# Three pieces of VectorE's instruction order moved inside a stage of a fused attention and expert kernel

## The reference

```python
# 1 delta-rule attention: q, k, v (4, 8, 768, 48), beta (4, 8, 768); per batch and head, over t:
k_n = k / (norm(k) + 1e-6)
y[t] = q[t] @ state
state += beta[t] * outer(k_n[t], v[t] - k_n[t] @ state)
# 2 gated layer: x (3072, 384), w_gate and w_val (384, 1536), w_out (1536, 384)
x = (sigmoid(x @ w_gate) * (x @ w_val)) @ w_out
# 3 top-1 routing among 8 experts, w1 (384, 1024), w2 (1024, 384)
logits = normalized(x) @ normalized(expert_emb).T / tau
e = argmax(logits); gate_w = softmax(logits)[e]
out = gate_w * (relu(x @ w1[e]) @ w2[e])
```

## Time and profile before

| | us |
|---|---|
| median of three runs | 1312.58 (1311.84 to 1313.44) |
| the profiled execution | 1311.84 |
| its span in the profile | 1310.2 |
| PE busy | 1269.6 (97%) |
| PE weight loads busy | 1036.0 (79%) |
| DVE busy | 633.8 (48%) |
| POOL busy | 462.8 (35%) |
| ACT busy | 406.9 (31%) |

### The profile page before, as it was taken

The page is one execution under the profiler, slowest core; times in us unless marked ns, Lnnn a source line. Parts: engine busy times, 40 slices in busy tenths (PEclk is TensorE's granted clock), DMA queues, the critical chain, the costliest instruction groups (busy, mean ns, idle before and its releaser), DMA issues.

```text
span 1310.2 us, 27998 instructions
## 1 busy us (share of the span) xinstructions
PE 1269.6 (97%) x11217; PEld 1036.0 (79%) x11217; DVE 633.8 (48%) x1512; ACT 406.9 (31%) x949; POOL 462.8 (35%) x525
## 2 busy tenths in 40 slices
PE   5888999999999999999999999999899999999998
PEld 3667999999999999999999999999455555555554
DVE  6765556656666666766666666533411111111111
ACT  3443333333433333334334343422111111111110
POOL 7545333334333433433333433323332222222220
PEclk9999999999999999999999999999999999999999
DMA  7332010020101021111111010033463223311000
GB/s 232 94 93 72 19 40 28 28 40 25 38 26 34 29 39 29 29 27 40 28 28 40 24 32 14 20 109 98 80 175 129 78 80 124 132 37 36 31 28 1
DMA packets 49118, 74.79 MB, mean 57 GB/s; under 512 B 8569, under 2 KB 37665, under 8 KB 48992
## 3 DMA queue, kind: packets, MB, share of 16 engines
q1 hardware_dynamic: 41504, 61.91, 16.5%
q0 software_dynamic: 7488, 11.08, 2.8%
HBM read 61.59 MB, written 12.75 MB: 57 GB/s over the span
## 4 chain that ended last, share of the span: by engine, by line
PE 88%; POOL 3%; DMA 3%; issue 3%; DVE 2%; ACT 1%; POOLq 0%; SPq 0%; DVEq 0%
PE ps L1259 25%; PE ps L1271 12%; PE ps L1495 11%; PE ps L1485 11%; PE ps L1131 3%; PE ps L1220 3%; PE ps L1228 3%; PE ps L1156 2%; PE ps L1148 2%; PE ps L1159 2%; PE ps L1226 2%; PE ps L1504 2%; PE ps L1115 2%; PE ps L1203 1%; DMA gates_dram<-gate,slot 1%
## 5 line engine op out<-in xcount | busy, mean ns | idle before, releaser
L1259 PE MATMUL ps<-xh,wgh 128*128 128x256 f32 x864 | 263.6, 305 | 0.7 <-issue 0.7
L1259 PE MATMUL ps<-xl,wgh 128*128 128x256 f32 x864 | 243.5, 282 | 0.0
L1259 PE MATMUL ps<-xh,wgl 128*128 128x256 f32 x864 | 242.8, 281 | 0.0
L411 POOL TENSOR_TENSOR gl<-sg,gh 128x256 fp32r<-128x256 f32 x144 | 105.7, 734 | 354.1 <-ACT gh L967 343.0
L1485 PE MATMUL ps<-W,xsT 128*128 x372 | 169.5, 605 | 2.1 <-ACT xsT L1094 1.2
L1259 PEld LDWEIGHTS ps<-xh,wgh 128*128 128x128 f32 x864 | 163.7, 189 | 7.9 <-issue 7.0
L1495 PE MATMUL ps<-W,hT 128*128 x496 | 165.2, 486 | 2.7 <-DVE hT L909 1.8
L642 DVE TENSOR_TENSOR MP<-ps,mE 128x512 f16<-128x512 f32 x126 | 87.2, 692 | 166.8 <-PE ps L1148 166.5
L1259 PEld LDWEIGHTS ps<-xl,wgh 128*128 128x128 f32 x864 | 164.3, 190 | 1.0 <-issue 1.0
L1259 PEld LDWEIGHTS ps<-xh,wgl 128*128 128x128 f32 x864 | 163.6, 189 | 0.0
L1495 PEld LDWEIGHTS ps<-W,hT 128*128 128x128 f32 x496 | 94.1, 190 | 75.2 <-issue 17.6
(11 more groups left out here) (203 smaller groups left out, 2354.0 us busy)
## 6 DMA issues: line engine op xcount, KB each, us to landing
W<-w_dram SPq DMA_DIRECT2D x16, 1536.0 KB, 11.8
betaT<-betaT_dram SPq DMA_DIRECT2D x48, 128.0 KB, 3.0
kin<-kv_dram SPq DMA_DIRECT2D x24, 192.0 KB, 3.2
kqT<-qT_dram SPq DMA_DIRECT2D x48, 96.0 KB, 2.6
vin<-kv_dram SPq DMA_DIRECT2D x24, 192.0 KB, 2.4
x_dram<-x2r SPq DMA_DIRECT2D x24, 192.0 KB, 2.0
stage<-w_gate_dram SPq DMA_DIRECT2D x6, 384.0 KB, 4.9
woT<-woT_dram SPq DMA_DIRECT2D x1, 2304.0 KB, 12.1
```

What stands on the lines that cost most here:

```text
L411: pool.tensor_tensor(gl[n % 2][:, :], gp[n % 2][:, :], gh[n % 2][:, :].bitcast(F32), ALU.subtract).then_inc(gl_ok, 1)
L1259: mm = pe.matmul(ps[n % 2][:, kind * TB:(kind + 1) * TB], w[:, kind, a, cs], v[m % 2][:, a, :], start=(a == 0 and x == 0), stop=(a == KT - ...
```

## The change

Three moves in the order of DVE's instructions in `body`; no instruction is added or removed, and no other engine's code changes.

```diff
             if moe:
                 gated(n + 2)
-            if g is not None:
-                level_mask(g, 4)
             if cg is not None and cg < NG - B:
                 state_update(cg)
+            if g is not None:
+                level_mask(g, 4)
             if moe:
                 gated(n + 3)
             if routed(s) is not None:
                 choose(routed(s))
-            if g is not None:
-                level_mask(g, 5)
-            if cg is not None:
-                x_low(cg)
             if settled(s) is not None:
                 gate_a(settled(s))
                 gate_b(settled(s))
             if g is not None:
+                level_mask(g, 5)
+            if cg is not None:
+                x_low(cg)
+            if settled(s) is not None:
+                gate_c(settled(s))
+            if g is not None:
                 level_mask(g, 6)
             if nxt is not None:
                 scaled_transposed(nxt)
             if moe:
                 gated(n + 4)
-            if settled(s) is not None:
-                gate_c(settled(s))
```

More of the change, by code:

```diff
@@ L773, in body @@
                 gated(n + 2)
+            if cg is not None and cg < NG - B:
+                state_update(cg)
             if g is not None:
                 level_mask(g, 4)
-            if cg is not None and cg < NG - B:
-                state_update(cg)
             if moe:
@@ L781, in body @@
                 choose(routed(s))
+            if settled(s) is not None:
+                gate_a(settled(s))
+                gate_b(settled(s))
             if g is not None:
@@ L786, in body @@
             if settled(s) is not None:
-                gate_a(settled(s))
-                gate_b(settled(s))
+                gate_c(settled(s))
             if g is not None:
```

## The result

The changed kernel took 1322.79 us (median of 5 runs, 1320.36 to 1326.16), the kernel before 1313.22 us (5 runs, 1311.84 to 1316.59). The ratio is 1.0073, with a 95% interval of 1.0051 to 1.0095: slower by 6.7 to 12.5 us. A second measurement of the same two kernels, later, gave 1.0076 (1.0051 to 1.0102). The direction was as predicted, and so were the place and the mechanism of the largest cost. The time was not: 1322.79 lies above 1319.2 and just outside the range of 1315 to 1322.

What follows compares the result with a forecast made beforehand. PE was taken to bound stages 3 to 23, so only its waits add time. Nine stops of 0.74 us (6.7 us), all other terms 0, on the 1312.58 us median gave 1319.2 us; range 1315 to 1322.

Steps and rivals of the forecast that it cites:

- What bounds the kernel, and where the slack is: Stages 3 to 23: only PE waits add time; DVE's level 5 mask can be 0.20 us late before PE stops.
- `gate_a` and `gate_b`: nine places, 0.74 each: Level 5 mask, even stages 6 to 22: chain meets POOL's subtraction, mask 0.94 us late, PE stops 0.74; 6.7 us in all.
- Rival 1: Level 5 mask: the chain delays it but the port does not matter; 9 x 0.18 = 1.6 us, 1314.2; chance 11%.
- `key_transposes` met "with 0.02 to spare": PE behind the late level 5 mask: x_low is seen at 459.01, transposes due at 459.03, so no second stall.
- rival 3: Late mask stops PE twice, at level_products and key_transposes; 0.5 us more each, 9 x 1.24 = 11.2, 1323.8; chance 7%.
- The state update at 0: State update ahead of the level 4 mask, s=3 to 20: fits DVE's idle time, no PE wait goes away, cost 0.
- Its signs of being wrong: L562 takes its usual 0.16, chain ends before PE's level_masked 5, waits at L1108, or waits in the odd stages.
- `gate_c` and the tail at 0: gate_c before the level 6 mask hides in DVE idle time; tail s=24 and 26 has 0.88 us margin; cost 0.
- The sum: Whole kernel: 6.7 us added to 1311.84 gives 1318.5; laid on the three-run median 1312.58, 1319.2 us, slower by 0.5%.

Runs made afterwards that it cites:

- kernel with reciprocals: Changed kernel with the second root step replaced by three one-operand reciprocals in settled stages; 1.0017 against the kernel before.
- chain-cut kernel with the old state order: Changed kernel with only six of nine gate instructions before the level 5 mask and state update back behind the level 4 mask; 1.0003 against the kernel before.
- last four experiments: Whole change again 1.0076; gate_a ahead of gated(n+3) 1.0014; one more chain instruction 1.0100; six-instruction chain with state update back 1.0003; kernel before 1316.29 us.

## Why the prediction was right in kind and wrong in time

- **What bounds the kernel, and where the slack is.** Right. PE had next to no idle time in stages 3 to 23 (one pause of 0.7 us, in stage 7), and the usable slack of the level 5 mask was 0.20 us: a mask 2.13-1.74=0.39 late cost 0.18 to 0.19, one 0.94 late cost 0.73.
- **`gate_a` and `gate_b`: nine places, 0.74 each.** Right, to 0.01. The collision came where it was worked out (the second `L562`, 0.03 behind POOL's start). The Trainium skill, "SBUF — State Buffer", section "Who interferes with whom", has two-input DVE instructions block on a GpSimd instruction that reads SBUF and was issued first; the trace agrees, 0.72 us against 0.17 for the one-input reciprocals beside the same POOL instruction. The prediction's own wording, that an instruction which reads two SBUF tensors waits, leaves out the TENSOR_SCALAR with one input that waited as well (0.60 in s=24). Rival 1 (0.18 each) is what the kernel with reciprocals does, not this one.
- **`key_transposes` met "with 0.02 to spare".** Wrong by a little. It waited 0.07 to 0.08 for `x_low` at each of the nine places: `L1108` starts 465.12-464.59=0.53 us after `L1156`, where it was 458.26-457.81=0.45 without a wait. That is 0.7 us in all, a small form of rival 3, and the prediction's sum had it at 0. The margin of 0.02 rested on matmul starts; the weight loads start earlier against the groups before them, and it is they that wait.
- **The state update at 0.** This is the step that failed. The prediction took the level 4 mask to wait for PE "as it did", gave stage 7 alone "at most about 0.2 us in all", and then 0. It asked what waits for the state update and not what stands behind it in DVE's queue when its signal is late. Stage 7 alone made PE wait 0.55 to 0.62 us in every kernel with the new order, and stages 9 and 17 came on top, whose late signals (1.04 and 1.02 us) stood in the trace of before too. Cost: 1.6 us by the waits, 1.4 us timed (-0.4 to 3.2). The waits are shown; their worth in time is not clear of zero.
- **Its signs of being wrong.** The prediction named four, and two came true: waits at `L1108` and waits in the odd stages. They belong to the two terms above that it put at 0.
- **`gate_c` and the tail at 0.** Right: the chain-cut kernel with the old state order has the early `gate_c` and gives 1.0003, and the tail (last `L1156` to last `L1303`) took 73.92 us in the changed kernel and 73.94 before.
- **The sum.** 9 x (0.73 + 0.07) + 1.4 = 8.6 us, a ratio of 1.0065; measured 1.0073 and 1.0076, with intervals from 1.0051 up. The forecast had 6.7 us. It missed by 3.6 us. Of these, 1.9 are cost that it left out (state update and `key_transposes`, less 0.1 at the nine places). Another 0.6 come from laying it on a median of three runs, 1312.58, where five gave 1313.22. The last 1.0 no run puts down to anything; it is within the interval. The kernel before took 1316 to 1317 us on the chips of the experiments. The range ended at 1322, hardly beyond the forecast's own 1320.5, although its bounds came from a single profiled execution.

The profiled execution of the changed kernel was 1325.37 us, above the median, and its trace 13.5 us longer than that of before. By the starts of the first and last weight load of `L1156` from stage 3 on, of the last `L1303` and the first `L1485`, it had 3.3 us more up to stage 3, 8.7 in stages 3 to 23, 0.0 in the tail and 1.5 in the experts. Only the 8.7 can be the change's: the tail took the same time, the code before stage 3 and of the experts is the same, the second execution of the same kernel had 0.6 more up to stage 3, and the experts took 370.6 to 374.5 us in the ten traces.

## What to carry to other kernels

When small work is put ahead of something that the bound engine waits for, measure the hole it goes into (here 1.40 us between `gated(n+3)` and the mask, plus 0.20 of slack) and look at what the neighbour engine does in it: 0.18 us of overrun became 0.73 because the last instructions met a POOL operation 0.03 us after its start. An order that equals the producer's order is not free by that: in a queue, the least urgent instruction should stand behind the most urgent one, because a late signal then delays only itself. And a cost of some 7 us on a kernel that scatters by 10 us (1312.49 to 1322.42 in the last four experiments) is found by counting waits at a repeated place, not by comparing busy shares.

## What the runs showed of the hardware that I had not expected

- A RECIPROCAL of 128x2 elements from SBUF to SBUF was not held up by POOL (0.17 us beside a running subtraction). A SCALAR_TENSOR_TENSOR of the same size was, until 0.01 us after POOL's end (0.72 us), and so was a TENSOR_SCALAR that reads one tensor, until 0.03 us after it (0.60 us).
- PE's completion signal for the state update came 0.26 to 4.25 us after the modelled end of the matmuls at the same three stages (7, 9, 17) of all ten kernels, where 0.02 to 0.03 is usual. All ten also have a pause in PE's own starts in stage 7, for which the profile names no releaser: 0.68 us before, 0.45 in the changed kernel, 2.2 with only the state update moved.
- The kernel before ran at 1313, 1317 and 1316 us on the three occasions; the ratio of the change came out the same on two of them to 0.0003. As each interval is 0.002 wide to either side, that closeness is luck.
